# Tails in transfers of their own, rotated on DVE, and a new first order, in an attention kernel with two feed-forward layers behind it

## The chip, the cores and the metric

The kernel runs on one core of a Trainium2 chip. The metric is the device time of the whole program in microseconds (us). A change of 0.2% is 2.2 us here.

## The reference, cut to what matters

```python
def rotate(x):                       # q and k, [4, 8, 576, 64], float32
    x1, x2 = x[..., :32], x[..., 32:]
    return concatenate([x1 * cos - x2 * sin, x1 * sin + x2 * cos], axis=-1)
scores = matmul(rotate(q), rotate(k).T) / sqrt(64)
scores = scores - max(scores, axis=-1)
attn = exp(scores) / (sum(exp(scores)) + 1e-9)
x = matmul(attn, v)                  # heads side by side: [2304, 512]
x = (s * relu(x @ w_in) ** 2 + b) @ w_out          # 512 -> 2048 -> 512
h = x @ w2_in
out = (h * sigmoid(1.702 * h)) @ w2_out
```

## The kernel before, in words

The 32 heads are taken in 16 pairs. A head has 576 rows: 512 of them ("mains", NM = 4 tiles of 128) and 64 more ("tails"). The tails of the two heads of a pair share one tile, head 0 on partitions 0 to 63 and head 1 on 64 to 127. To keep float32 accuracy a matrix product is made of a high part (rounded to fp32r) and a low part (the rest), so each operand is split by ACT (high) and DVE (low).

A job is named kind, head and tile, and after the @ the pair: S01@2 is tile 1 of head 0 of pair 2. For each pair these jobs follow one another:

- load: SP issues the transfers of q and k into `raw` (L431 mains, L433 tails, which come as one transfer of [2, 64, 64] for q and one for k).
- rot: POOL rotates a head (L388 two products, L398 and L399 a difference and a sum), and adds one to `rotated`. A load waits until the rotation before it has read `raw`.
- prep: PE transposes the rotated head into PSUM (L679, L681). qk: ACT writes the high part (L781). klo: DVE writes the low part (L858).
- qcopy, kcopy: SP moves the parts between partitions (L456, L461). S00 of a pair with p > 0 waits for its kcopy.
- S, ST: PE makes a tile of scores (L579) and the tile of the tails (L594). max: DVE (L805, L811). exp: ACT (L713, L720).
- X, XQ, XT: PE transposes the exponentials (L605, L615, L631). hi: ACT. lo: DVE. PV: PE multiplies by V (L651), which takes V's parts from POOL (V, L518, and vlo, L522). eps, inv, IT, put, get, finish: the sums' reciprocals and the last scaling.

PE, ACT, DVE, POOL and SP each run their jobs strictly in the order of a list written out by hand: `PE_FIRST` and its like for about the first three pairs, then `PE_ORDER` and its like, repeated with a step of a pair. `FIRST_SLOTS` says which PSUM banks a job takes; a job whose bank is still to be read waits for its reader. The feed-forward layers follow (L956, L984).

Pair 0 has a path of its own. Its q and k go to `raw_0` (a part of buffer E), mains of head 0, tails, mains of head 1 (L483, L485, L487), and ACT issues the rotation tables' mains, their tails (L786, one transfer of [2, 64, 32] for each table) and the identity that PE transposes with (L787). DVE rotates the mains in four groups, q and k of head 0 and q and k of head 1 (`first_products` L405, two instructions; `first_sums` L416, L418); POOL rotates the tails in the same way. The first groups add to `first_rotated`, the tails to `first_tails`. Then `prep_first` (L666, L668) transposes, ACT makes the high parts (L771, L773), and DVE the low ones in `qk_first` (L840, L842). POOL starts rot0@1 after `first_rotated` has come to 4, which is all four groups.

Of the kernel before, what the change touches and what calls it, by code (L numbers as in the profile page):

```python
# [30 lines left out]
def fused_kernel(nc, q, k, v, w1_in, w1_out, w_s, w_b, w2_in, w2_out,  # L31
# [66 lines left out]
    SP_FIRST = order("load0@2 qcopy0@1 load1@2 kcopy0@1 qcopy1@1 kcopy1@1 load0@3 load1@3 qcopy0@2 qcopy1@2 kcopy0@2 "
                     "loadv0@1 kcopy1@2 load0@4 load1@4 qcopy0@3 qcopy1@3 load0@5 kcopy0@3 put@0 kcopy1@3 loadv1@1 "
                     "loadv0@2 qcopy0@4 get@0 kcopy0@4 load1@5 load0@6 put@1 loadv1@2 qcopy1@4 loadv0@3 get@1")  # L100
    FIRST_SLOTS = [0, 0, 0, 1, 3, 0, 2, 1, 3, 0, 5, 0, 3, 1, 2, 0, 1, 3, 1, 0, 3, 2, 1, 1, 3, 4, 5, 0, 3, 2, 0, 1, 4,
                   5, 7, 1, 0, 1, 2, 0, 3, 1, 0, 3, 2, 1, 0, 3, 0, 3, 2, 7, 2, 3, 0, 2, 6, 7, 2, 3, 0, 1, 7, 2, 0, 3,
# [1038 lines left out]
```

## Time and profile before

| | us |
|---|---|
| median of 3 runs | 1118.81 (1118.38 to 1119.59) |
| the profiled execution's own time | 1119.24 |
| its span | 1117.4 |
| PE busy in the span | 1090.4 |
| DVE, ACT, POOL busy | 553.5, 500.8, 247.4 |

The span is the time from the first to the last instruction in the trace, here 1.84 us less than that execution's own time. Matrix multiplications are pipelined, so that PE's busy time is not PE at its peak, but a stretch in which PE isn't busy is one in which nothing is computed there.

### The profile page before, as it was taken

What the parts mean: (1) busy time and instruction counts of PE and PEld (TensorE: products, weight loads), DVE (VectorE), ACT (ScalarE), POOL (GpSimd) and SP (SyncE); (2) the same over time, 40 slices, a digit from 0 to 9 for tenths busy, and PEclk for the clock granted to TensorE, in tenths of its full rate; (3) what the DMA queues carried; (4) which work ended last, traced back from release to release, by engine and by line L of the source; (5) the groups of instructions that cost most, each with busy time, mean ns of one, the idle gap of its engine ahead of it and who ended that gap; (6) DMA issues with size and microseconds to landing.
All of it is one profiled execution on the core that took longest, in us unless ns stands there. A gap on an engine that the chain in (4) does not pass through costs nothing.

```text
span 1117.4 us, 16936 instructions
## 1 busy us (share of the span) xinstructions
PE 1090.4 (98%) x6522; PEld 1036.1 (93%) x6522; DVE 553.5 (50%) x885; ACT 500.8 (45%) x1031; POOL 247.4 (22%) x276
## 2 busy tenths in 40 slices
PE   4899999999999999999999999999999999999998
PEld 4899999999999999999999999999999999999997
DVE  6888888898866333333333356532332323333222
ACT  4888788878755332232332345422322222222222
POOL 6878878895720000000000000000000000000000
PEclk9999999999999999999999999999999999999999
DMA  4555454553243100000000014200000000000000
GB/s 109 126 147 145 128 152 130 147 138 91 69 132 125 37 1 1 1 1 1 1 1 1 1 57 133 76 1 1 29 1 29 1 15 15 1 29 1 29 1 29
DMA packets 59187, 59.47 MB, mean 53 GB/s; under 512 B 13780, under 2 KB 46820, under 8 KB 59108
## 3 DMA queue, kind: packets, MB, share of 16 engines
q1 hardware_dynamic: 58272, 57.90, 18.6%
q8 instruction: 52, 0.85, 0.3%
q10 hardware_dynamic: 836, 0.49, 0.1%
q14 instruction: 27, 0.22, 0.1%
HBM read 35.88 MB, written 4.79 MB: 36 GB/s over the span
## 4 chain that ended last, share of the span: by engine, by line
PE 90%; DVE 4%; ACT 3%; DMA 1%; issue 1%; POOL 1%; SPq 0%; ACTq 0%; POOLq 0%; DVEq 0%
PE psum L956 36%; PE psum L984 36%; PE psum L651 7%; PE psum L605 4%; PE psum L579 4%; ACT E L713 2%; DVE negmax L805 1%; PE psum L681 1%; DVE osum L835 1%; DVE Xlo L815 1%; PE psum L615 0%; PE psum L631 0%; DMA sin<-in_k_sin_dram 0%; PE psum L679 0%; DVE QK L858 0%
## 5 line engine op out<-in xcount | busy, mean ns | idle before, releaser
L956 PE MATMUL psum<-xhi,Wlo 128*128 128x384 f32 x768 | 257.8, 336 | 0.0
L956 PE MATMUL psum<-xhi,Whi 128*128 128x384 f32 x768 | 257.6, 335 | 0.0
L956 PE MATMUL psum<-xlo,Whi 128*128 128x384 f32 x768 | 257.2, 335 | 0.0
L956 PEld LDWEIGHTS psum<-xhi,Whi 128*128 128x128 f32 x768 | 144.2, 188 | 4.2
L956 PEld LDWEIGHTS psum<-xlo,Whi 128*128 128x128 f32 x768 | 144.1, 188 | 4.1
L956 PEld LDWEIGHTS psum<-xhi,Wlo 128*128 128x128 f32 x768 | 144.1, 188 | 0.0
L937 DVE SCALAR_TENSOR_TENSOR glo<-act,sb_sb,ghi 128x384 fp32r<-128x384 f32 x96 | 59.4, 619 | 145.4 <-ACT ghi L924 145.4
L924 ACT ACTIVATE ghi<-act,sb_sb 128x384 fp32r<-128x384 f32 x96 | 59.2, 617 | 157.7 <-PE psum L984 150.3
L940 DVE TENSOR_TENSOR glo<-act,ghi 128x384 fp32r<-128x384 f32 x96 | 53.6, 559 | 152.0 <-ACT ghi L926 152.0
L984 PE MATMUL psum<-ghi,Whi 128*128 128x384 f32 x384 | 128.3, 334 | 0.0
L984 PE MATMUL psum<-glo,Whi 128*128 128x384 f32 x384 | 128.3, 334 | 0.0
L984 PE MATMUL psum<-ghi,Wlo 128*128 128x384 f32 x384 | 128.3, 334 | 0.0
L926 ACT CAST ghi<-act 128x384 fp32r<-128x384 f32 x96 | 49.3, 514 | 157.0 <-PE psum L984 157.0
L934 DVE TENSOR_TENSOR act<-psum,act 128x384 f32<-128x384 f32 x96 | 53.5, 558 | 124.1 <-ACT act L920 124.1
L984 PE MATMUL psum<-Wlo,ghi 128*128 128x512 f32 x288 | 113.9, 396 | 0.0
L984 PE MATMUL psum<-Whi,glo 128*128 128x512 f32 x288 | 113.7, 395 | 0.0
L984 PE MATMUL psum<-Whi,ghi 128*128 128x512 f32 x288 | 111.9, 389 | 0.0
L920 ACT ACTIVATE act<-psum 128x384 f32<-128x384 f32 x96 | 47.2, 492 | 129.6 <-PE psum L956 129.6
L713 ACT ACTIVATE E<-psum,negmax 128x576 f32<-128x576 f32 x128 | 94.7, 745 | 13.6 <-DVE negmax L805 13.3
L805 DVE TENSOR_REDUCE negmax<-psum 128x1 f32<-128x576 f32 x128 | 91.2, 752 | 14.7 <-PE psum L579 14.1
L932 DVE SCALAR_TENSOR_TENSOR act<-act,sb_sb 128x384 f32<-128x384 f32 x96 | 60.3, 628 | 76.4 <-ACT act L918 76.4
L579 PE MATMUL psum<-QK,Q 128*128 128x320 f32 (+1 forms) x512 | 86.3, 309 | 9.1 <-ACT E L713 6.9
(107 smaller groups left out, 1844.4 us busy)
## 6 DMA issues: line engine op xcount, KB each, us to landing
Q<-QK SPq DMA_DIRECT2D x60, 144.0 KB, 3.1
QK<-QK SPq DMA_DIRECT2D x30, 288.0 KB, 3.4
wraw<-in_moe_w_in_dram SPq DMA_DIRECT2D x32, 256.0 KB, 2.9
wraw<-in_moe_w_out_dram SPq DMA_DIRECT2D x32, 256.0 KB, 3.1
vraw<-in_v_dram SPq DMA_DIRECT2D x32, 128.0 KB, 2.3
raw<-in_q_dram SPq DMA_DIRECT2D x30, 128.0 KB, 2.9
raw<-in_k_dram SPq DMA_DIRECT2D x30, 128.0 KB, 2.8
inv_row<-inv_dram SPq DMA_DIRECT2D x16, 144.0 KB, 2.9
```

The source lines that it names most:

```text
L579: mm = pe.matmul(ps[:, a:b], Q[h][p % 2][:, at:at + P], QK[h][p % 2][:, part, c:c + b - a], start=part == 0, stop=part == 1)
L651: mm = pe.matmul(ps[:, a:b], V[h][:, j, :, :].rearrange("p a d -> p (a d)"), x, start=j == 0 and n == 0, stop=j == NM and n == 1, skip_gro ...
L713: act.activation(E[p % 2][:, j, h, :], row(banks("S", p, h, j), h), ACT.Exp, bias=negmax[p % 2][:, c:c + 1], accum_out=sums[p % 2][:, c:c ...
L805: dve.tensor_reduce(negmax[p % 2][:, c:c + 1], row(banks("S", p, h, j), h), AX_X, ALU.max, negate=True).then_inc(max_done, 1)
L924: act.activation(ghi[n % 2][:], a[:], ACT.Identity, bias=sb_sb[:, 1:2]).then_inc(g_hi, 1)
L926: act.copy(ghi[n % 2][:], a[:]).then_inc(g_hi, 1)
L932: dve.scalar_tensor_tensor(a[:], a[:], sb_sb[:, 0:1], a[:], ALU.mult, ALU.mult).then_inc(g_done, 1)
L934: dve.tensor_tensor(a[:], hps(n), a[:], ALU.mult).then_inc(g_done, 1)
L937: dve.scalar_tensor_tensor(glo[n % 2][:], a[:], sb_sb[:, 1:2], ghi[n % 2][:].bitcast(F32), ALU.add, ALU.subtract).then_inc(g_lo, 1)
L940: dve.tensor_tensor(glo[n % 2][:], a[:], ghi[n % 2][:].bitcast(F32), ALU.subtract).then_inc(g_lo, 1)
L956: mm = pe.matmul(hps(n), w[i][:, kt * P:(kt + 1) * P], x[C % 2][:, kt, :], start=kt == 0 and j == 0, stop=kt == KT - 1 and j == 2)
L984: mm = pe.matmul(dst, lhsT, rhs, start=i == 0 and j == 0, stop=i == NF - 1 and j == 2)
```

## The change

1. **Transfers.** The tails of pairs 0 and 1 (q and k) and the tails of the tables go as one transfer for each half of the partitions: 64 rows each, 16 transfers in place of 8. From pair 2 on the tails are as before.
2. **Who rotates the tails of pair 0.** DVE does, after head 0's q and k and before head 1's q. POOL's six instructions for it go, and so do `first_tails` and `tails_step`. `first_rotated` now counts five groups: q0, k0, tails, q1, k1. PE's `prep_first(0)` waits for 3 of them, `prep_first(1)` for 4 and 5. POOL's wait before rot0@1 is still for 4.
3. **Low parts.** `qk_first(0)` on DVE comes ahead of the group k1 (it was the first job of `DVE_FIRST`).
4. **ACT** loads its table and makes its first small exponential before it waits for the rotation tables.
5. **Orders.** All five first lists and the slots are new. On PE ST@0 comes before S02@0, prep0@1 before ST@0, X01@0 before S13@0, and prep0@3 and prep1@3 come ahead of PV0@0, where prep1@3 came after S03@2 and ST@2.

```diff
-    PE_FIRST = order("prep0@0 prep1@0 S00@0 S01@0 S02@0 prep0@1 S03@0 ST@0 S10@0 prep1@1 X00@0 S11@0 S12@0 S13@0 S00@1 "
-                     "prep0@2 S01@1 S02@1 S03@1 S10@1 prep1@2 S11@1 ST@1 XQ@0 XT@0 X01@0 X02@0 S12@1 S13@1 X03@0 IT@0 "
-                     "X10@0 X11@0 X12@0 X13@0 prep0@3 PV0@0 S00@2 S01@2 S02@2 S03@2 ST@2 prep1@3 S10@2 S11@2 S12@2 "
+    PE_FIRST = order("prep0@0 S00@0 S01@0 prep1@0 prep0@1 ST@0 S02@0 S03@0 S10@0 prep1@1 S11@0 S12@0 X00@0 X01@0 S13@0 "
+                     "S00@1 S01@1 S02@1 S03@1 prep0@2 prep1@2 X02@0 X03@0 S10@1 S11@1 ST@1 IT@0 XT@0 XQ@0 S12@1 "
+                     "prep0@3 X10@0 X11@0 X12@0 S13@1 X13@0 prep1@3 PV0@0 ST@2 S00@2 S01@2 S02@2 S03@2 S10@2 S11@2 "
...
+    ACT_FIRST = order("qk0@0 exp00@0 qk1@0 qk0@1 exp01@0 expT@0 exp02@0 qk1@1 exp03@0 exp10@0 hi00@0 hi01@0 exp11@0 "
...
+    DVE_FIRST = order("klo0@0 max00@0 max01@0 klo1@0 klo0@1 maxT@0 max02@0 max03@0 max10@0 klo1@1 max11@0 max12@0 "
...
+    POOL_FIRST = order("rot0@1 rot1@1 V0@0 rot0@2 rot1@2 eps@0 vlo0@0 rot0@3 rot1@3 V1@0 V0@1 vlo1@0 eps@1 rot0@4 rot1@4 "
...
+    SP_FIRST = order("load0@2 qcopy0@1 load1@2 kcopy0@1 qcopy1@1 kcopy1@1 load0@3 load1@3 loadv0@1 qcopy0@2 qcopy1@2 "
...
-                def tails(t, p):
-
-                    return t[2 * p:2 * p + 2, MAIN:S, :]
+                def tails(rows, t, p, apart):
+
+                    if apart:
+                        for h in range(2):
+                            yield rows[rows_of(h), :], t[2 * p + h, MAIN:S, :]
+                    else:
+                        yield rows, t[2 * p:2 * p + 2, MAIN:S, :]
...
-                            sp.dma_start(to[:, w, NM, :], tails(t, p)).then_inc(qk_in[h], 16)
+                            for dst, src in tails(to[:, w, NM, :], t, p, p == 1):
+                                sp.dma_start(dst, src).then_inc(qk_in[h], 16)
...
-                        pool.wait_ge(qk_in[h], (64 if h == 0 else 32) * p)
+                        pool.wait_ge(qk_in[h], 96 + 64 * (p - 1) if h == 0 else 32 * p)
...
-                pool.wait_ge(tab_tails_in, 32)
-                pool.wait_ge(first_tails_in, 32)
-                for w in range(2):
-                    first_products(pool, w, NM, NM + 1, slice(NM, NT), tails_step)
-                first_sums(pool, 4, NM, NM + 1, None, tails_step, first_tails)
+                pool.wait_ge(tab_tails_in, 64)

                 pool.wait_ge(first_rotated, 4)
...
                 def prep_first(h):
-                    pe.wait_ge(first_tails, 1)
...
-                        pe.wait_ge(first_rotated, 2 * h + w + 1)
+                        pe.wait_ge(first_rotated, 3 if h == 0 else 4 + w)
...
-                    act.dma_start(tab[:, NM, :], src[0:TAIL, NM, :].unsqueeze(0).broadcast_to([2, TAIL, HALF])).then_inc(tab_tails_in, 16)
+                    for h in range(2):
+                        act.dma_start(tab[rows_of(h), NM, :], src[0:TAIL, NM, :]).then_inc(tab_tails_in, 16)
                 act.dma_start(id_sb[:], ident).then_inc(id_in, 16)
+                act.wait_ge(cleared, 1)
+                act.activation(negmax[0][:], sums[0][:], ACT.Exp)
...
-                for n, (first, w) in enumerate(((0, 0), (0, 1), (NM + 1, 0), (NM + 1, 1))):
-                    dve.wait_ge(first_in[n], 16)
-                    first_products(dve, w, first, first + NM, slice(0, NM), first_step)
-                    first_sums(dve, 2 * n + 2, first, first + NM, w, first_step, first_rotated)
+                dve.wait_ge(first_in[0], 16)
+                first_tiles(0, 0, NM, (0,), slice(0, NM))
+                dve.wait_ge(first_in[1], 16)
+                first_tiles(1, 0, NM, (1,), slice(0, NM))
+                dve.wait_ge(tab_tails_in, 64)
+                dve.wait_ge(first_tails_in, 64)
+                first_tiles(2, NM, NM + 1, (0, 1), slice(NM, NT))
+                dve.wait_ge(first_in[2], 16)
+                first_tiles(4, NM + 1, TILES, (0,), slice(0, NM))
+                qk_first(0)
+                dve.wait_ge(first_in[3], 16)
+                first_tiles(5, NM + 1, TILES, (1,), slice(0, NM))
```

`first_tiles` makes the products of the groups that it is given and then their difference and sum, six instructions for the tails and four for each of the others.

## Rows read from the trace of the kernel before

**Rows 1.** The page's busy time of each engine, share of the span and instructions.
```profile
PE 1090.4 (98%) x6522; PEld 1036.1 (93%) x6522; DVE 553.5 (50%) x885; ACT 500.8 (45%) x1031; POOL 247.4 (22%) x276
```

**Rows 2.** Stretches: length, PE, PEld, DVE, ACT, POOL busy, clock, DMA share, GB/s.
```profile
12.00:26.00 14.00, 11.32 (x69) 10.12 (x69) 9.62 (x14) 9.00 (x19) 12.98 (x12) 1.00 0.28 73
26.00:29.00 3.00, 2.68 (x11) 2.38 (x11) 1.92 (x3) 1.94 (x5) 2.86 (x3) 0.51 0.82 197
29.00:45.00 16.00, 14.04 (x106) 12.74 (x105) 13.75 (x21) 14.13 (x33) 12.41 (x15) 0.99 0.64 159
45.00:90.00 45.00, 42.76 (x329) 40.31 (x329) 38.06 (x59) 34.72 (x79) 37.29 (x40) 1.00 0.48 121
```

**Rows 3.** The chain that ended last, from 0 to 60 us: start, length, what.
```profile
3.07 5.17 DMA sin<-in_k_sin_dram
...
8.47 1.93 POOL E L405 x4
```

**Rows 4.** The stretch 8.3 to 9.6 us, columns as in rows 2.
```profile
8.30:9.60 1.30, 0.00 (x0) 0.00 (x0) 1.27 (x4) 1.28 (x1) 1.13 (x3) 1.00 0.15 39
```

**Rows 5.** DMA issues in order of time, and line L442 by itself (ns).
```profile
1.67 1.36 ACTq L786 DMA_DIRECT2D cos<-in_k_cos_dram  x1
7.15 1.98 SPq L431 DMA_DIRECT2D raw<-in_q_dram  x1
L442 SPq DMA_DIRECT2D vraw<-in_v_dram x3: 493/528/802, 10.1 to 39.1; - x3
DMA to landing us min/median/max: 2.0/2.3/2.6
```

**Rows 6.** DVE's, then POOL's instructions in order of time: start, length, what.
```profile
5.24 0.42 DVE L405 TENSOR_TENSOR E<-E,cos 128x256 f32<-128x256 f32 x1
6.37 0.42 DVE L418 TENSOR_TENSOR E<-E 128x256 f32<-128x256 f32 x1
8.07 0.43 DVE L405 TENSOR_TENSOR E<-E,cos 128x256 f32<-128x256 f32 x1 [1.28 <-DMA E<-in_q_dram]
9.67 0.54 DVE L405 TENSOR_TENSOR E<-E,cos 128x256 f32<-128x256 f32 x1
10.13 0.54 DVE L405 TENSOR_TENSOR E<-E,sin 128x256 f32<-128x256 f32 x1
9.89 0.50 POOL L405 TENSOR_TENSOR E<-E,sin 128x64 f32<-128x64 f32 x1
10.95 0.63 POOL L418 TENSOR_TENSOR E<-E 128x128 f32<-128x128 f32 x1
```

**Rows 7.** PE's and DVE's instructions in order of time, from 11.8 us on.
```profile
11.83 0.45 PE L666 MATMUL psum<-id_sb,E 128*128 128x128 f32 x1 [11.83 <-POOL E L418]
14.90 0.76 DVE L842 TENSOR_TENSOR QK<-psum,QK 128x576 fp32r<-128x576 f32 x1
17.52 2.08 DVE L805 TENSOR_REDUCE negmax<-psum 128x1 f32<-128x576 f32 x3
20.39 1.30 PE L594 MATMUL psum<-QK,Q 128*128 128x256 f32 x10
23.84 0.82 DVE L858 SCALAR_TENSOR_TENSOR QK<-psum,qk_scale,QK 128x576 fp32r<-128x576 f32 x1 [0.20 <-ACT QK L781]
```

**Rows 8.** SP's, POOL's and PE's instructions around pair 3's rotation, in order of time.
```profile
16.79 0.33 SPq L431 DMA_DIRECT2D raw<-in_q_dram  x1
29.84 1.39 SPq L431 DMA_DIRECT2D raw<-in_q_dram  x1
21.56 1.55 POOL L388 TENSOR_TENSOR byc<-raw,cos 128x640 f32<-128x640 f32 x1 [0.64 <-DMA raw<-in_k_dram]
36.23 1.55 POOL L388 TENSOR_TENSOR byc<-raw,cos 128x640 f32<-128x640 f32 x1 [3.35 <-DMA raw<-in_k_dram]
45.18 0.74 POOL L399 TENSOR_TENSOR rot<-bys,byc 128x256 f32<-128x256 f32 x1
43.58 0.36 PE L651 MATMUL psum<-Xhi,V 128*128 128x256 f32 x1
```

More of the change, by code:

```diff
@@ L78, in fused_kernel @@
     BANK_ORDER = (6, 0, 7, 1, 2, 3, 4, 5)
-    PE_FIRST = order("prep0@0 prep1@0 S00@0 S01@0 S02@0 prep0@1 S03@0 ST@0 S10@0 prep1@1 X00@0 S11@0 S12@0 S13@0 S00@1 "
[4 rows of a table removed]
-    ACT_FIRST = order("qk0@0 qk1@0 exp00@0 exp01@0 qk0@1 exp02@0 exp03@0 qk1@1 expT@0 hi00@0 exp10@0 exp11@0 exp12@0 "
[5 rows of a table removed]
-    DVE_FIRST = order("klo0@0 klo1@0 max00@0 max01@0 max02@0 klo0@1 max03@0 maxT@0 max10@0 klo1@1 lo00@0 max11@0 "
[5 rows of a table removed]
-    POOL_FIRST = order("rot0@1 rot1@1 rot0@2 rot1@2 V0@0 eps@0 V1@0 vlo0@0 rot0@3 vlo1@0 rot1@3 eps@1 V0@1 vlo0@1 rot0@4 "
-                       "rot1@4 rot0@5 eps@2 V1@1 V0@2 vlo1@1 vlo0@2 rot1@5 finish@0 V1@2 vlo1@2 rot0@6 finish@1")
@@ L98, in fused_kernel @@
[L98 to L102, printed above, removed]
+    PE_FIRST = order("prep0@0 S00@0 S01@0 prep1@0 prep0@1 ST@0 S02@0 S03@0 S10@0 prep1@1 S11@0 S12@0 X00@0 X01@0 S13@0 "
[4 rows of a table added]
@@ new lines, in fused_kernel @@
+    ACT_FIRST = order("qk0@0 exp00@0 qk1@0 qk0@1 exp01@0 expT@0 exp02@0 qk1@1 exp03@0 exp10@0 hi00@0 hi01@0 exp11@0 "
[5 rows of a table added]
+    DVE_FIRST = order("klo0@0 max00@0 max01@0 klo1@0 klo0@1 maxT@0 max02@0 max03@0 max10@0 klo1@1 max11@0 max12@0 "
[5 rows of a table added]
+    POOL_FIRST = order("rot0@1 rot1@1 V0@0 rot0@2 rot1@2 eps@0 vlo0@0 rot0@3 rot1@3 V1@0 V0@1 vlo1@0 eps@1 rot0@4 rot1@4 "
+                       "V1@1 vlo0@1 vlo1@1 eps@2 rot0@5 rot1@5 V0@2 finish@0 V1@2 vlo0@2 vlo1@2 rot0@6 finish@1")
+    SP_FIRST = order("load0@2 qcopy0@1 load1@2 kcopy0@1 qcopy1@1 kcopy1@1 load0@3 load1@3 loadv0@1 qcopy0@2 qcopy1@2 "
+                     "kcopy0@2 load0@4 kcopy1@2 qcopy0@3 qcopy1@3 load1@4 kcopy0@3 kcopy1@3 loadv1@1 load0@5 put@0 "
+                     "qcopy0@4 qcopy1@4 loadv0@2 load1@5 get@0 loadv1@2 put@1 kcopy0@4 load0@6 load1@6 kcopy1@4 "
+                     "loadv0@3 get@1 qcopy0@5")
@@ L103, in fused_kernel @@
+    FIRST_SLOTS = [0, 1, 0, 0, 1, 2, 0, 3, 1, 2, 0, 2, 7, 2, 3, 0, 2, 1, 3, 0, 2, 1, 0, 1, 3, 2, 2, 3, 1, 2, 1, 7, 6,
+                   0, 2, 1, 1, 3, 1, 3, 0, 2, 1, 3, 0, 2, 1, 3, 0, 4, 1, 6, 7, 0, 1, 2, 0, 3, 2, 7, 6, 2, 0, 1, 2, 3,
                    1, 0, 2, 7, 6, 1, 0, 2, 1, 0]
@@ L197, in fused_kernel @@
         first_rotated = sem("first_rotated")
-        first_tails = sem("first_tails")
-        tails_step = sem("tails_step")
         first_t = sem("first_t")
@@ L484, in attention_sync @@
                 for w, t in enumerate((q_h, k_h)):
-                    sp.dma_start(group(raw_0, NM, NM + 1)[:, w, 0, :], tails(t, 0)).then_inc(first_tails_in, 16)
+                    for dst, src in tails(group(raw_0, NM, NM + 1)[:, w, 0, :], t, 0, True):
+                        sp.dma_start(dst, src).then_inc(first_tails_in, 16)
                 for w, t in enumerate((q_h, k_h)):
@@ L785, in attention_scalar @@
                 for tab, src in ((cos, k_cos), (sin, k_sin)):
-                    act.dma_start(tab[:, NM, :], src[0:TAIL, NM, :].unsqueeze(0).broadcast_to([2, TAIL, HALF])).then_inc(tab_tails_in, 16)
+                    for h in range(2):
+                        act.dma_start(tab[rows_of(h), NM, :], src[0:TAIL, NM, :]).then_inc(tab_tails_in, 16)
                 act.dma_start(id_sb[:], ident).then_inc(id_in, 16)
+                act.wait_ge(cleared, 1)
+                act.activation(negmax[0][:], sums[0][:], ACT.Exp)
                 act.wait_ge(tabs_in, 32)
-                act.wait_ge(tab_tails_in, 32)
+                act.wait_ge(tab_tails_in, 64)
                 for tab, twice in ((cos, cos_2), (sin, sin_2)):
                     act.copy(twice[:], tab[:, :, :].unsqueeze(2).broadcast_to([P, NT, 2, HALF])).then_inc(tabs_twice, 1)
-                act.wait_ge(cleared, 1)
-                act.activation(negmax[0][:], sums[0][:], ACT.Exp)
                 act.wait_ge(scale_set, 1)
@@ L855, in qk_low @@
                     if p == 0:
-                        return qk_first(h)
+                        return qk_first(1) if h == 1 else None
                     dve.wait_ge(qk_hi, 2 * p + h + 1)
@@ L863, in attention_vector, with first_tiles @@
                 dve.wait_ge(tabs_in, 32)
-                for n, (first, w) in enumerate(((0, 0), (0, 1), (NM + 1, 0), (NM + 1, 1))):
-                    dve.wait_ge(first_in[n], 16)
-                    first_products(dve, w, first, first + NM, slice(0, NM), first_step)
-                    first_sums(dve, 2 * n + 2, first, first + NM, w, first_step, first_rotated)
+                def first_tiles(n, first, end, ws, tab):
+                    for w in ws:
+                        first_products(dve, w, first, end, tab, first_step)
+                    first_sums(dve, 2 * n + 2 * len(ws), first, end, ws[0] if len(ws) == 1 else None, first_step, first_rotated)
+                dve.wait_ge(first_in[0], 16)
[10 more added lines that the diff above has]
+                first_tiles(5, NM + 1, TILES, (1,), slice(0, NM))
                 dve.wait_ge(cleared, 1)
```

24 rows, old and new, of tables (ACT_FIRST, DVE_FIRST, PE_FIRST) are left out of this document.

## The prediction, made before the change was run

> **What bounds the kernel now.** I read the page first: PE is busy 98% of the span, so the time is PE's work plus what PE stands idle [rows 1]. The change adds and removes no work on PE; it can only shift idle time, and there are 27.0 us of it (1117.4 - 1090.4). Next I read the busy time by stretches. PE starts at 11.83 [rows 7], idles 2.7 us from 12 to 26, 0.3 from 26 to 29, 2.0 from 29 to 45 and 2.2 from 45 to 90 [rows 2]. So 19 of the 27 us lie ahead of 90 us, and the change touches only that part. The granted clock matters too: it is 0.51 from 26 to 29, the level of 1.2 GHz, after PE had waited in the stretch before [rows 2]. Third, the chain of waits shows what holds the start: the tables' tails, issued at 3.07, land at 8.24, POOL takes them up at 8.47 [rows 3], and PE starts when POOL's L418, begun at 10.95 [rows 6], is done. Last, the timelines of POOL, SP and PE around 30 to 46 us, since the first order moves jobs there [rows 8].
>
> **The transfers.** From 8.3 to 9.6 us, with only the tails still in flight (pair 1's behind pair 0's), the DMA share is 0.15 at 39 GB/s [rows 4]: 2.4 of 16 engines. A transfer of [2, 64, ...] seems to run on about two engines. The nearest row for the new form is L442, V's tails, 64 rows from one head: issue 0.53, landing 2.3 us after the issue starts [rows 5]. In the new kernel SP issues two mains from 0.74 at 0.45 each and four tails at 0.53, the last from 3.2; ACT's last tail of a table also starts at about 3.2. Both land at about 5.5 to 6. Issues that took 1.36 and 1.98 [rows 5] could add up to 2 us; DVE has work until 6.8 [rows 6], which hides a landing at 6 and 0.8 us more.
>
> The row L442 speaks for the spread by itself. The Trainium skill, page "DMA: Bandwidth & Descriptors", section "Rules for kernel authors", says the opposite of what this change does: two transfers to disjoint halves of the partitions are not worth it, since they serialize on the same engines, and one should be used. By it the tails would land no sooner than 8.2; the trace has 2.3 us for a half and some 5 for the whole, so the row disagrees for this shape; rival E has that outcome.
>
> **The tails on DVE.** Six instructions of 64 or 128 columns. Below they cost nothing beyond the order (DVE waits 1.28 us for q1 anyway, up to 8.07 [rows 6]); above, six at the 0.42 of 256 columns, 2.5 us. Four of 256 columns take 1.5 us in a row (5.24 to 6.79 [rows 6]), and these have a quarter or half of the columns, so I take 1.1 us for the six. DVE goes 6.8 to 7.9, PE starts at about 8.0, **3.8 us earlier**. q1 is rotated from 7.9 to 9.4. In before DVE ended the first low parts at 15.66, 3.83 after PE's start [rows 7]; now 11.85. S00@0 can run then.
>
> **POOL against DVE.** This is where I think the lead is lost. POOL's rot0@1 waits for `first_rotated` 4, which was everything and is now only q1, at 9.4. Its data: four more issues stand ahead of its end on SP's queue (two tails of pair 0, two of its own), the last starts at about 7.1 to 8.1, and lands at 9.4 to 10.4. So rot0@1 starts at about 10.4, not 11.94, and the group k1, which comes after `qk_first(0)` at 11.85, runs beside it. In before DVE's instructions with two inputs in SBUF, which take 0.42 alone, take 0.54 and start every 0.46 while POOL rotates the tails; POOL's end at 10.39, DVE's at 10.21 and 10.67, so they alternate: 0.28 for DVE, 0.18 for POOL's 64 columns, and 0.31 for its 128 [rows 6]. Two bounds follow. If only a fixed 0.12 to 0.2 is lost, k1 takes 2.2 us and ends at 14.0. If each waits for the whole instruction of the other, k1's four instructions alternate with POOL's, of 1.5 us and twice about 0.8 (estimated for 320 columns from 0.74 for 256) [rows 8]: 11.9 to 12.2, 13.7 to 14.0, 14.8 to 15.1, 15.9 to 16.2; with another start of POOL the end is up to 17.1. Since POOL's turn grew from 0.18 to 0.31 as its columns doubled, I take 16.2. The Trainium skill, page "SBUF — State Buffer", section "Who interferes with whom", has it so: a VectorE instruction with two SBUF inputs and a GpSimd one that reads SBUF lock each other out for the whole instruction. By that rule k1 ends at 16.2 to 17.1, without it at 14.0; this trace shows it only for small POOL instructions.
>
> The first maximum is then made at 16.2 against 17.52 [rows 7], but DVE still owes the second head's low parts (1.5 us), which it had made by then. On this order: two maxima to 17.6, exp00 to 17.65, the second head's high parts on ACT to 18.9, its low parts to 19.85, klo0@1 to 20.6.
>
> **From there to the copies.** ST@0 takes 1.30 [rows 7], then S02, S03 and S10 (0.65 each) and prep1@1 (0.6): 23.7. With 0.75 for ACT and 0.8 for DVE, klo1@1 ends at 25.3, against 24.66 before [rows 7]. That is at full clock. But between 13.8 and 19.85 PE has little to do, and before the clock fell at 26 after a stretch with more work than that. At its start PE's transposes take 0.21 each up to about 15.4 and half of that later (the clock column shows 1.00 there, so I go by the durations), and from 26 to 29 the clock is 0.51: some 3 to 3.6 us at half rate each time. An estimate from these: 3.6 us at half rate from 19.85, which costs 1.8, klo1@1 at 27.1. The bounds are 25.3 and 27.1.
>
> **The load of pair 3 and prep1@3.** SP has load0@3 behind kcopy1@1, in both kernels. Before, it was issued at 29.84, and rot0@3 started at 36.23, after POOL had idled 3.35 us for it [rows 8]. From klo1@1's end to the issue it took 5.2 us, of which 0.75 for kcopy0@1 ahead of it, so 4.45 now: 29.75 or 31.55. From issue to rotation it is 6.4 us, or 4.8 as for pair 2 (16.79 to 21.56 [rows 8]): rot0@3 starts at 34.5 to 37.9. Both heads of pair 3 take 8.8 us (36.23 to 45.92, less 0.88 for vlo1@0 between them, which moves behind). Now prep1@3 stands ahead of PV0@0 on PE, and behind it waits everything PE has. Before, PE reached prep1@3 4.6 us after its rotation was done, and PV0@0 at 43.58 [rows 8]. The four combinations give rot1@3 done at 43.3, 44.9, 45.1 or 46.7 (29.75 or 31.55, plus 4.8 or 6.4, plus 8.8); with prep1@3 (0.6) PV0@0 starts at 43.9, 45.5, 45.7 or 47.3. Less the 0.6 of prep1@3, which is then done, PE is behind by -0.2, 1.4, 1.6 or 3.2 us. I take the mean, 1.5. From 45 us on PE is 95% busy [rows 2], so there is little to catch up with: of 2.2 us idle perhaps 0.1.
>
> The rest costs nothing: ACT's table load lies in its wait for the tables, and POOL's removed six instructions (3.1 us, 8.47 to 11.58 [rows 3, 6]) lay in a stretch where it now waits for pair 1's data.
>
> **The sum.** +1.5 - 0.1 = +1.4 us. Against the profiled execution 1119.24 + 1.4 = 1120.6; that execution was 0.4 above the median, and against the median 1118.81 the forecast is **1120.2**. A difference of 0.2%, 2.2 us, is about what a measurement tells from none.
>
> **The rivals.**
> - *A, the forecast*: the lead of 3.8 us goes to POOL and DVE locking each other and to the wait for prep1@3. -0.3 to +2.2 us. Chance 0.40.
> - *B, the same with the low clock and the slow landing*: +2.3 to +4, 1121.1 to 1122.8. It decides from klo1@1 ending after 26.1 where the landing takes 6.4. For it: the clock fell at 26 after less idle time. Against it: the landing may be 4.8. Chance 0.26.
> - *C, DVE isn't held up*: k1 ends at 14.0, 2.2 before A's, and all behind it moves with it at full clock: klo1@1 at 23.1, load0@3 at 27.6, PV0@0 at 41.8 to 43.4. PE leads by 0.8 to 2.4: 1116.4 to 1118.0. Chance 0.15, a third of it beyond 0.2%.
> - *D, the whole start is kept*: load0@3 is early enough that prep1@3 isn't late, and the new order loses nothing: -2.5 to -3.8, 1115.0 to 1116.3. Against it: POOL waited 3.35 us for this very load. Chance 0.13. It decides, beyond 0.2%, where klo1@1 ends before 23.3 with the landing in 4.8, before 21.7 with it in 6.4.
> - *E, the change of transfers does nothing* (the halves go on the same two engines one after the other: 4.6 us from issue to landing in place of 2.3, and two more issues): tails at 8.8, DVE through with them at 9.9, PE at 10.0, everything 2 us later than in A: about 1122. Chance 0.06.
>
> Slower by over 0.2%: B and most of E, and a little of A, 0.34. Faster: D, a third of C and errors in my hand count, 0.21. Within: 0.45. For 8 in 10 the range reaches from most of D to the middle of B: 1116.0 to 1122.4. A's own range is 1118.5 to 1121.0.
>
> **What would show it.** The transfers: DVE's wait before the tails is near nothing, and PE's first matmul starts at 8 to 8.5; at 10 or later would be E. The lock: the four instructions of k1 (L405, L416, L418) take about 1.5 us each or stand apart by that; at about 0.5 each in a row it is C. The clock: S tiles and ST@0 at half rate around 20 to 24. The load: POOL idle before rot0@3 on `raw`, and PE idle before L679 or L681 of prep1@3, just ahead of PV0@0, 1 to 4 us. The prediction is wrong if PE isn't idle there; then look whether load0@3 was issued before 28.

## The result, and the profile after

| | before | after |
|---|---|---|
| median, us (8 runs of each) | 1118.52 (1117.88 to 1119.59) | 1121.12 (1120.55 to 1122.4) |
| the profiled execution's own time | 1119.24 | 1121.25 |
| its span | 1117.4 | 1119.4 |

The ratio of the times is 1.0025, with an interval of 1.0014 to 1.0036: **2.6 us slower**, with 1.6 to 4.0 us as the interval: slower is clear, whether by more than 0.2% (2.2 us) is not quite. The forecast was 1120.2. By its account (+1.4) it was 1.2 us short, and the time lies at the lower end of rival B.

The page's busy times after, to be read against [rows 1]:

```profile
PE 1093.5 (98%) x6522; PEld 1037.7 (93%) x6522; DVE 556.9 (50%) x891; ACT 500.0 (45%) x1031; POOL 244.4 (22%) x270
```

PE has the same 6522 instructions and is busy 3.1 us longer, so it ran slower somewhere; its idle time is 25.9 us against 27.0. The sum is the 2.0 us of the span. Where they lie shows the busy time by stretches: first after, in the stretches of [rows 2] and then up to the first matmul of PV0@0 and from it on (columns as in rows 2):

```profile
12.00:26.00 14.00, 11.28 (x51) 9.91 (x51) 11.03 (x13) 5.02 (x11) 10.94 (x10) 1.00 0.32 78
26.00:29.00 3.00, 2.08 (x15) 1.88 (x16) 2.35 (x4) 2.26 (x6) 2.74 (x3) 1.00 0.46 98
29.00:45.00 16.00, 13.09 (x96) 11.21 (x95) 13.17 (x21) 14.52 (x34) 11.77 (x13) 1.00 0.65 154
45.00:90.00 45.00, 43.49 (x330) 40.59 (x328) 38.47 (x60) 34.48 (x79) 37.97 (x41) 1.00 0.49 127
...
8.06:46.43 38.37, 29.83 (x177) 25.74 (x178) 30.89 (x44) 24.25 (x54) 28.73 (x28) 1.00 0.52 123
...
46.43:1119.40 1072.97, 1063.65 (x6348) 1011.91 (x6346) 521.73 (x832) 473.51 (x973) 214.63 (x229) 1.00 0.18 50
```

The last two stretches for the kernel before, from PE's start to its PV0@0 and from there on:

```profile
11.83:43.58 31.75, 26.78 (x173) 24.00 (x173) 23.88 (x36) 23.80 (x54) 26.97 (x27) 0.95 0.51 127
...
43.58:1117.40 1073.82, 1063.62 (x6351) 1012.05 (x6350) 522.84 (x833) 474.81 (x974) 216.40 (x230) 1.00 0.18 50
```

PE starts 3.77 us earlier, but needs 38.37 us to PV0@0 in place of 31.75: 3.05 more busy (0.6 of it prep1@3, which now stands ahead; the rest is more time at half rate, by the durations below) and 3.57 more idle (8.54 against 4.97). So it comes to PV0@0 2.85 us late, and makes up 0.85 from there to the end. Between 12 and 26 us PE is as busy as before, 11.28 us, but for 51 instructions in place of 69.

DVE's instructions after, in order of time (start, length, what), which answer to [rows 6] and [rows 7]:

```profile
6.76 0.22 DVE L404 TENSOR_TENSOR E<-E,cos 128x64 f32<-128x64 f32 x1
...
11.81 1.67 DVE L404 TENSOR_TENSOR E<-E,cos 128x256 f32<-128x256 f32 x1
13.40 1.08 DVE L404 TENSOR_TENSOR E<-E,sin 128x256 f32<-128x256 f32 x1
14.52 0.97 DVE L415 TENSOR_TENSOR E<-E 128x256 f32<-128x256 f32 x1
15.41 1.48 DVE L417 TENSOR_TENSOR E<-E 128x256 f32<-128x256 f32 x1
16.82 1.41 DVE L807 TENSOR_REDUCE negmax<-psum 128x1 f32<-128x576 f32 x2
...
26.78 0.82 DVE L861 SCALAR_TENSOR_TENSOR QK<-psum,qk_scale,QK 128x576 fp32r<-128x576 f32 x1 [0.43 <-ACT QK L782]
```

POOL's after, the first ones and rot0@3:

```profile
10.15 1.54 POOL L387 TENSOR_TENSOR byc<-raw,cos 128x640 f32<-128x640 f32 x1 [8.61 <-DMA raw<-in_k_dram]
11.64 1.55 POOL L387 TENSOR_TENSOR bys<-raw,sin 128x640 f32<-128x640 f32 x1
13.28 0.93 POOL L397 TENSOR_TENSOR rot<-byc,bys 128x320 f32<-128x320 f32 x1
14.17 1.04 POOL L398 TENSOR_TENSOR rot<-bys,byc 128x320 f32<-128x320 f32 x1
15.35 1.26 POOL L387 TENSOR_TENSOR byc<-raw,cos 128x512 f32<-128x512 f32 x1
...
36.83 1.57 POOL L387 TENSOR_TENSOR byc<-raw,cos 128x640 f32<-128x640 f32 x1 [2.91 <-DMA raw<-in_k_dram]
```

The tails come at once (nothing waited for at 6.76, PE starts at 8.06). Then the lock: POOL's instructions end at 13.19, 14.21, 15.21 and 16.61, and the four of k1 on DVE, which take 0.42 alone, at 13.48, 14.48, 15.49 and 16.89, each 0.27 to 0.29 us behind POOL's. The first maximum is at 16.82, against 17.52, and klo1@1 ends at 27.60, against 24.66.

PE's after (the first bracket is what it waited for), and SP's issue of load0@3:

```profile
8.06 0.45 PE L667 MATMUL psum<-id_sb,E 128*128 128x128 f32 x1 [8.06 <-DVE E L417]
...
12.04 2.26 PE L580 MATMUL psum<-QK,Q 128*128 128x256 f32 x8 [1.61 <-DVE QK L844]
...
20.68 2.42 PE L595 MATMUL psum<-QK,Q 128*128 128x256 f32 x10 [0.81 <-DVE QK L844]
22.91 2.51 PE L580 MATMUL psum<-QK,Q 128*128 128x256 f32 x12
...
27.65 0.80 PE L580 MATMUL psum<-QK,Q 128*128 128x320 f32 x4 [0.92 <-DVE QK L861]
...
45.91 0.33 PE L680 MATMUL psum<-id_sb,rot 128*128 128x128 f32 x1 [0.41 <-POOL rot L398]
...
46.43 0.37 PE L652 MATMUL psum<-Xhi,V 128*128 128x256 f32 x1
```

```profile
31.12 0.58 SPq L434 DMA_DIRECT2D raw<-in_q_dram  x1
```

One thing fits the forecast's picture and one stands against it. ST@0 takes 2.42, where it took 1.30 before [rows 7], so PE runs at 1.2 GHz there, as the prediction's sign for the clock had it. But the wait ahead of prep1@3, which was to be 1 to 4 us, is 0.41. The other waits from 26 to 46 us are spread: 0.92 at 27.65 for klo1@1 and others of 0.16 to 1.06.

### The profile page after: what moved, and what is told of

Same layout as the page of the kernel before. It is cut to its first block, busy times and chain, and to the rows that moved or that the text cites. A ratio compares the mean times of both kernels' runs of the same rounds, so it can differ in the third digit from the quotient of the medians.

```text
span 1119.4 us, 16941 instructions
## 1 busy us (share of the span) xinstructions
PE 1093.5 (98%) x6522; PEld 1037.7 (93%) x6522; DVE 556.9 (50%) x891; ACT 500.0 (45%) x1031; POOL 244.4 (22%) x270
## 4 chain that ended last, share of the span: by engine, by line
PE 92%; DVE 3%; ACT 2%; POOL 1%; issue 1%; DMA 0%; ACTq 0%; POOLq 0%
PE psum L972 36%; PE psum L1000 36%; PE psum L652 8%; PE psum L606 4%; PE psum L580 4%; ACT E L714 2%; PE psum L682 1%; DVE negmax L807 1%; DVE osum L837 1%; PE psum L632 1%; PE psum L616 1%; PE psum L680 0%; PE psum L595 0%; DVE E L404 0%; POOL bys L387 0%
```

## The experiments

Twelve kernels were run, each beside the kernel before on the same chip. Times are medians; the difference is to the kernel before in the same comparison (1118.45 to 1118.70). Line numbers in rows are those of each kernel's own file.

| run | median (lowest to highest), us | difference | ratio, interval |
|---|---|---|---|
| 1. k1 ahead of the low parts | 1118.97 (1117.62 to 1119.44) | +0.5 | 1.0003, 0.9994 to 1.0012 |
| 2. POOL waits for k1 | 1119.56 (1119.32 to 1120.71) | +1.1 | 1.0011, 1.0002 to 1.002 |
| 3. the transfers alone | 1116.44 (1115.9 to 1118.23) | -2.0 | 0.9983, 0.9974 to 0.9992 |
| 4. prep1@3 behind PV0@0 | 1124.51 (1122.46 to 1124.86) | +6.1 | 1.0046, 1.0033 to 1.006 |
| 5. the old orders | 1121.21 (1120.89 to 1123.05) | +2.6 | 1.0025, 1.0015 to 1.0035 |
| 6. old orders, 1 and 2 together | 1117.02 (1116.84 to 1117.2) | -1.6 | 0.9985, 0.9976 to 0.9994 |
| 7. PE kept busy to 18 us | 1120.87 (1120.07 to 1122.19) | +2.3 | 1.0022, 1.0014 to 1.0031 |
| 8. the transfers undone | 1121.79 (1121.41 to 1122.92) | +3.2 | 1.003, 1.0018 to 1.0041 |
| 9. PE kept busy up to ST@0 | 1120.63 (1119.78 to 1122.1) | +2.1 | 1.0018, 1.0009 to 1.0027 |
| 10. old orders and k1 first | 1116.58 (1115.94 to 1117.0) | -1.9 | 0.9983, 0.9974 to 0.9992 |
| 11. as 3, tails apart for pairs 0 to 4 | 1116.56 (1116.06 to 1118.24) | -1.9 | 0.9984, 0.9975 to 0.9993 |
| 12. old orders, POOL waits for k1 | 1119.56 (1118.89 to 1120.62) | +0.9 | 1.0008, 0.9999 to 1.0017 |

Each interval reaches about 0.1%, 1.1 us, to either side. Those of run 1 and the change don't meet, nor do those of run 10 with run 1 or with run 5. Runs 2, 7, 8, 9 and 12 overlap with the kernel that they vary, and run 4 just does. What is said of the size of their effects rests on medians and on the rows of one profiled execution of each.

### Runs 1 and 2: taking k1 away from POOL's rotation

Run 1 puts the group k1 back ahead of the first low parts:

```diff
-                qk_first(0)
                 dve.wait_ge(first_in[3], 16)
                 first_tiles(5, NM + 1, TILES, (1,), slice(0, NM))
+                qk_first(0)
```

> The changed kernel with one thing undone: the group k1 on DVE comes before the first low parts again. Theory 1 (POOL and DVE keep each other out, so k1 beside rot0@1 ends at 16.8 and all behind it is late, at half clock): k1 now runs at 9.3 to about 11, at most its last instruction beside POOL's first (from 10.15); S00@0 starts at about 12.6 to 13, the first maximum at about 13.5 in place of 16.8, klo1@1 ends at 24 or earlier in place of 27.6, and the kernel is 2 to 4 us faster than the changed one (1117 to 1119). Theory 2 (the new order's waits for pair 3's rotation set the time): less than 1 us faster than the changed one, PE waits at prep1@3 for what is gained.

Run 2 leaves DVE's order and lets POOL start rot0@1 only behind k1:

```diff
-                pool.wait_ge(first_rotated, 4)
+                pool.wait_ge(first_rotated, 5)
```

> The changed kernel, but POOL waits for all five groups before rot0@1. Theory 1: k1's four instructions take 0.42 each again (1.5 us in all, done at 13.3), the first maximum is made at 13.3, but rot0@1 starts at 13.4 in place of 10.15, 3.2 us later, so prep0@1 (18.6 before) stays where it is and only what doesn't hang on it is early: 0.5 to 2 us faster than the changed kernel. If POOL's start doesn't slow k1 (theory 2), k1 still takes 5 us and the kernel is slower by 1 to 3 us, since the rotations are later.

Run 1 is 2.15 us faster than the change. Three of k1's instructions now take 0.42; the last still meets POOL's first. DVE's last one, the first maximum and klo1@1, and POOL's first, in run 1:

```profile
10.42 1.75 DVE L417 TENSOR_TENSOR E<-E 128x256 f32<-128x256 f32 x1
...
15.32 1.62 DVE L807 TENSOR_REDUCE negmax<-psum 128x1 f32<-128x576 f32 x2 [1.58 <-PE psum L580]
...
24.24 0.82 DVE L861 SCALAR_TENSOR_TENSOR QK<-psum,qk_scale,QK 128x576 fp32r<-128x576 f32 x1 [0.57 <-ACT QK L782]
```

```profile
10.15 1.75 POOL L387 TENSOR_TENSOR byc<-raw,cos 128x640 f32<-128x640 f32 x1 [8.60 <-DMA raw<-in_k_dram]
```

One instruction of 0.42 that starts 0.27 after POOL's becomes 1.75 and ends 0.27 behind it (12.17 against 11.90). With klo1@1 done at 25.06, PV0@0 comes at 43.94, though prep1@3 still stands ahead of it. PE's S00@0 and S01@0, ST@0 and the three tiles behind it, in run 1:

```profile
13.89 2.26 PE L580 MATMUL psum<-QK,Q 128*128 128x256 f32 x8 [3.47 <-DVE QK L844]
...
19.51 1.37 PE L595 MATMUL psum<-QK,Q 128*128 128x256 f32 x10 [1.31 <-DVE QK L844]
20.72 1.84 PE L580 MATMUL psum<-QK,Q 128*128 128x256 f32 x12
```

Not all of the gain is the lock. ST@0 starts 1.2 us earlier than in the change, and it and the tiles behind it are at full rate, 1.37 and 1.84 in place of 2.42 and 2.51, which is 1.7 us more. On the other side PE waits 3.47 us for the first low parts, so that S00@0 starts at 13.89 and not at 12.6 to 13 as expected, and klo1@1 ends at 25.06 and not at 24.

In run 2 k1 takes 0.42 for each instruction and the first maximum is at 13.44, 3.4 us before the change's. But rot0@1 starts at 13.65 in place of 10.15, and PE waits for it:

```profile
18.49 0.33 PE L680 MATMUL psum<-id_sb,rot 128*128 128x128 f32 x1 [2.46 <-POOL rot L398]
```

klo1@1 ends at 25.80 (27.60 in the change). ST@0 is at half rate there (2.43). So the lock is real and costs time, but taking it away by making POOL late gives back 1.6 us of it, no more.

### Runs 3, 8 and 11: the transfers

Run 3 is the kernel before with only the 16 transfers in halves: POOL still rotates the tails, and every order is as before.

```diff
-                    sp.dma_start(group(raw_0, NM, NM + 1)[:, w, 0, :], tails(t, 0)).then_inc(first_tails_in, 16)
+                    for dst, src in tails(group(raw_0, NM, NM + 1)[:, w, 0, :], t, 0, True):
+                        sp.dma_start(dst, src).then_inc(first_tails_in, 16)
...
-                    act.dma_start(tab[:, NM, :], src[0:TAIL, NM, :].unsqueeze(0).broadcast_to([2, TAIL, HALF])).then_inc(tab_tails_in, 16)
+                    for h in range(2):
+                        act.dma_start(tab[rows_of(h), NM, :], src[0:TAIL, NM, :]).then_inc(tab_tails_in, 16)
...
```

> The kernel before with only the 16 tails' transfers of 64 rows. If they spread over the DMA engines, the tails land at about 6 in place of 8.2, POOL rotates them at 6 to 8.5 (alternating with DVE), q1 is not waited for, PE starts at 9 to 9.5 in place of 11.83, and since all engines start 2 to 2.5 us earlier with the same orders, the kernel is 1.5 to 2.5 us faster than before (1116 to 1117). If halves serialize: PE starts at 11.5 or later and the time is that of before.

Run 8 is the change with the old single transfers; its diff is the reverse of this one, with the waits where the change has them. Run 11 is run 3 with `p == 1` made `1 <= p <= 4` for the pairs whose tails go apart.

> The changed kernel with the eight tails' transfers of before. Tails land at 8.2, DVE rotates them at 8.3 to 9.3, q1 after that to 10.8; PE starts at 9.5 in place of 8.06. POOL's rot0@1 then starts at 11 to 12 in place of 10.15, k1 runs beside it from about 13.3. All is 1 to 2 us later than in the changed kernel: 1 to 2 us slower (1122 to 1123). If the transfers are worth nothing here: the same time as the changed kernel.

> The kernel before with the tails' transfers apart for pairs 0 to 4 in place of 0 and 1. Loads of pairs 2 to 4 should land 0.5 to 1.5 us sooner, rot0@3 starts earlier. If PE's time hangs on them: 0.5 to 1 us faster than with pairs 0 and 1 alone (1115.5 to 1116). If not, as there, 1116.4, or a little more for two issues of 0.5 us more on SP's queue for each pair.

Run 3 gives 2.0 us, the largest gain of any one part. POOL's first instruction on the tails, PE's first and DVE's first maximum, in run 3:

```profile
6.03 0.32 POOL L405 TENSOR_TENSOR E<-E,cos 128x64 f32<-128x64 f32 x1 [4.48 <-DMA sin<-in_k_sin_dram]
```

```profile
9.17 0.44 PE L672 MATMUL psum<-id_sb,E 128*128 128x128 f32 x1 [9.17 <-POOL E L418]
```

```profile
15.05 2.08 DVE L812 TENSOR_REDUCE negmax<-psum 128x1 f32<-128x576 f32 x3
```

Against 8.47 [rows 3] for POOL, 11.83 and 17.52 [rows 7], these are 2.4, 2.7 and 2.5 us earlier. klo1@1 ends at 22.20 (24.66 before), load0@3 goes out at 27.40 (29.84 [rows 8]), and the span is 2.9 shorter, 1114.5. The lead is kept the whole way; the medians differ by 2.0. In run 8 DVE waits for the tables' tails, and PE starts 1.5 us after the change's 8.06, at 9.59:

```profile
8.28 0.23 DVE L404 TENSOR_TENSOR E<-E,cos 128x64 f32<-128x64 f32 x1 [1.42 <-DMA sin<-in_k_sin_dram]
```

The medians differ by only 0.7 us there (expected was 1 to 2). The profiled executions say something else: PV0@0 comes at 47.74 in place of 46.43, and the span is 1120.7 in place of 1119.4, so that 1.3 of the 1.5 us are still there at the end. Whether the transfers are worth 0.7 or 1.3 us inside the change isn't settled. Run 11 adds nothing to run 3 (the spans are both 1114.5), so tails of later pairs aren't waited for.

### Run 4: prep1@3 behind PV0@0

The theory was that PE loses its lead ahead of prep1@3. The lists keep the change's order but for this job and its readers on ACT and DVE, and the slots around it follow:

```diff
-                     "prep0@3 X10@0 X11@0 X12@0 S13@1 X13@0 prep1@3 PV0@0 ST@2 S00@2 S01@2 S02@2 S03@2 S10@2 S11@2 "
+                     "prep0@3 X10@0 X11@0 X12@0 S13@1 X13@0 PV0@0 prep1@3 ST@2 S00@2 S01@2 S02@2 S03@2 S10@2 S11@2 "
-                      "expT@1 hiT@0 hiQ@0 qk0@3 exp12@1 hi10@0 hi11@0 hi12@0 hi13@0 qk1@3 exp13@1 evac0@0 expT@2 "
+                      "expT@1 hiT@0 hiQ@0 qk0@3 exp12@1 hi10@0 hi11@0 hi12@0 hi13@0 exp13@1 evac0@0 qk1@3 expT@2 "
-                      "lo02@0 lo03@0 loT@0 max12@1 loQ@0 klo0@3 lo10@0 lo11@0 lo12@0 lo13@0 klo1@3 max13@1 sum0@0 "
+                      "lo02@0 lo03@0 loT@0 max12@1 loQ@0 klo0@3 lo10@0 lo11@0 lo12@0 lo13@0 max13@1 sum0@0 klo1@3 "
-                   0, 2, 1, 1, 3, 1, 3, 0, 2, 1, 3, 0, 2, 1, 3, 0, 4, 1, 6, 7, 0, 1, 2, 0, 3, 2, 7, 6, 2, 0, 1, 2, 3,
+                   0, 2, 1, 3, 1, 0, 3, 1, 2, 0, 3, 0, 2, 1, 3, 0, 4, 1, 6, 7, 0, 1, 2, 0, 3, 2, 7, 6, 2, 0, 1, 2, 3,
```

> The changed kernel with prep1@3 (and its high and low part) behind PV0@0, and the slots of ST@2, S01@2 to S03@2 changed so that no job waits for it sooner. The trace of the changed kernel has PE idle for only 0.41 us before prep1@3, so I expect 0.3 to 0.6 us faster, within what can be measured. The prediction's own step (PE is held 1 us or more by rot1@3) would want 1 us or more.

It was **3.4 us slower** than the change, where 0.3 to 0.6 us faster was expected. PE comes to PV0@0 at 46.60 all the same (46.43 in the change), after a wait for DVE's low parts. It then meets a new wait, and part of the stretch behind it is at half rate. PE's instructions, and the stretch 54 to 58 us, in run 4:

```profile
46.60 0.35 PE L652 MATMUL psum<-Xhi,V 128*128 128x256 f32 x1 [0.61 <-DVE Xlo L817]
...
56.14 3.21 PE L580 MATMUL psum<-QK,Q 128*128 128x320 f32 x12 [1.31 <-ACT E L714]
```

```profile
54.00:58.00 4.00, 2.67 (x13) 2.45 (x13) 2.19 (x4) 2.81 (x8) 3.78 (x5) 0.78 0.88 228
```

So prep1@3 isn't what makes PE late at PV0@0. What the move costs comes behind PV0@0, by these rows; no run took it apart.

### Runs 5, 6, 10 and 12: the orders

Run 5 is the change with all five first lists and slots of the kernel before. Run 10 adds run 1's edit, run 12 run 2's, and run 6 both.

> The changed kernel with the five first orders and the slots of before; transfers, tails on DVE, low parts ahead of k1 and POOL's wait for four stay. If the group k1 beside POOL is what costs, this order suffers more: prep1@0, ahead of S00@0, needs k1 (done at about 16.8), so S00@0 starts at about 17.5 in place of 15.89 before: 1 to 3 us slower than before (1119.5 to 1121.5). If the new orders are what costs, it is 2 to 3 us faster than before, like the transfers alone.

> The same with the old orders, k1 ahead of the low parts, and POOL waiting for all five groups, so that DVE's rotations never run beside POOL's. PE starts at 8.05, k1 is done at 10.8, S00@0 starts at about 12.1 (15.89 before), the first maximum at 13.7 (17.52), POOL's rot0@1 at 10.9 (11.94). If a start without that overlap is kept by the old orders: 2 to 3.8 us faster than before (1114.7 to 1116.5), at least as fast as the transfers alone. If POOL's chain of rotations and loads (1.1 us earlier) sets the gain: 1 us.

> The changed kernel with the old orders and k1 ahead of the low parts, POOL waiting for four groups. Only k1's last instruction meets POOL's first (10.15 to 11.7), which costs DVE 1.3 us and gives POOL 1.0 us against the run where it waited for five. If POOL's rotations set the pace there (PE waited 1.18 and 0.97 us for them), this is 0.3 to 1 us faster than that run (1116 to 1116.7); if DVE sets it, 0.5 to 1.3 us slower.

> The changed kernel with the old orders, low parts still ahead of k1, and POOL waiting for all five groups: it differs from the run with the old orders alone (1121.2) only in that POOL's rotation doesn't run beside k1. If the overlap is what costs there: k1's four instructions take 0.42 each and end at 13.4 in place of 16.9, the first maximum is made at about 16 in place of 19.7, POOL's rot0@1 starts at 13.5 in place of 10.2 and ends at 18.4, and the time is 2 to 3.5 us less (1117.7 to 1119.2). If it is the place of the low parts ahead of k1, whatever POOL does: 1120.5 to 1121.5 still.

With the old orders S00@0 stands behind prep1@0, and so behind k1. PE's wait for it and DVE's first maximum in run 5:

```profile
16.98 0.48 PE L666 MATMUL psum<-id_sb,E 128*128 128x128 f32 x1 [5.41 <-DVE E L416]
```

```profile
19.69 2.08 DVE L806 TENSOR_REDUCE negmax<-psum 128x1 f32<-128x576 f32 x3
```

The first maximum is 2.9 us behind the change's, yet klo1@1 ends at 26.84, 0.8 us before the change's, and the time is the same. DVE's rows in run 10, for comparison with run 1's:

```profile
10.53 1.76 DVE L416 TENSOR_TENSOR E<-E 128x256 f32<-128x256 f32 x1
...
15.33 0.76 DVE L806 TENSOR_REDUCE negmax<-psum 128x1 f32<-128x576 f32 x1
...
21.66 0.82 DVE L860 SCALAR_TENSOR_TENSOR QK<-psum,qk_scale,QK 128x576 fp32r<-128x576 f32 x1 [0.20 <-ACT QK L781]
```

The first maximum is at the same time in both (15.33, 15.32), but klo1@1 ends at 22.48 with the old orders and at 25.06 with the new ones, where the second head's preps stand behind S01@0 and its low parts behind two maxima. The medians differ by 2.4 us. PE's S00@0 to S02@0 in run 10, to be read against the 3.47 of run 1:

```profile
13.99 3.13 PE L579 MATMUL psum<-QK,Q 128*128 128x256 f32 x12 [0.33 <-DVE QK L843]
```

With the old orders PE makes prep1@0 (10.32 and 12.34) while it waits for the first low parts; with the new ones it stands idle and makes it from 15.95 on. So the second head's low parts are made at 13.88 to 15.41 in run 10 and at 17.84 to 19.37 in run 1, and ST@0 waits 1.31 us for them there. The corners, as differences to the kernel before:

| | old orders | new orders |
|---|---|---|
| k1 ahead of the low parts | -1.9 (run 10) | +0.5 (run 1) |
| low parts first, POOL waits for k1 | +0.9 (run 12) | +1.1 (run 2) |
| low parts first, POOL starts beside k1 | +2.6 (run 5) | +2.6 (the change) |

With k1 first, whether POOL waits for it too makes 0.4 us (run 6, 1117.02, against run 10, 1116.58), which is within the intervals. In run 6 all four instructions take 0.42, but PE then waits 1.18 and 0.97 us for POOL's rotation, so one lock of 1.3 us costs no more than the later start. Run 6 was expected to be at least as fast as run 3 and wasn't.

Run 12 came between what its two theories said. k1 is done at 13.41, 1.1 us later than in run 10, but rot0@1 starts at 13.73, 3.4 us later (10.32), and PE waits for it:

```profile
18.60 0.33 PE L679 MATMUL psum<-id_sb,rot 128*128 128x128 f32 x1 [1.23 <-POOL rot L397]
```

Together with a second wait of 0.99 behind it that puts klo1@1 at 25.16, against 22.48 in run 10 and 26.84 in run 5.

### Runs 7 and 9: the half rate

Both add transposes to PE that write the same values again, so that PE doesn't stand idle ahead of ST@0. Run 7 repeats prep1@0's q part seven times and puts 8 transposes ahead of S00@0. Run 9 also repeats its k part three times and puts 8 ahead of ST@0, as soon as DVE has read the bank. Its diff against run 7:

```diff
-                        for _ in range(7 if (h, w) == (1, 0) else 1):
+                        for _ in range(7 if (h, w) == (1, 0) else 3 if (h, w) == (1, 1) else 1):
...
+                    if p == 0:
+                        pe.wait_ge(low_read, 2)
+                        for n in range(8):
+                            pe.transpose(psum[2][:, ROW[0] + n % NM * P:ROW[0] + (n % NM + 1) * P], rotated_tile(NM + 1, NM + 1 + NM, n % NM, 0), id_sb[:])
...
```

> The changed kernel with 38 transposes more on PE, which write again what prep1@0 writes, in the idle time from 10.4 to 12 and 15.4 to 16.9 us; nothing else is changed. If PE's half rate up to 24 us costs (the low clock's share of the forecast): ST@0 takes 1.3 us in place of 2.42 and the three S tiles behind it 2.0 in place of 2.5, klo1@1 ends at 25.8 to 26.3 in place of 27.6, and the kernel is 1 to 2 us faster than the changed one. If the clock is of no account there, the time is the same.

> As the run before with repeated transposes, and more of them: the keys' part of prep1@0 three times in all, and eight ahead of ST@0, as soon as DVE has read the bank. The run before moved the half rate to 21 to 24.5 us and so didn't take it out of ST@0 and S02 to S10; here PE stands idle less than 0.6 us at a time up to ST@0. If it then stays at full rate: ST@0 takes 1.3 us, the three S tiles 2.0, klo1@1 ends at 25.5 to 26.3 (27.6 in the changed kernel), and the time falls by 1 to 2 us against the changed kernel if the half rate is worth that, or not at all if the load of pair 3 and DVE set it anyway.

ST@0 in run 7:

```profile
20.70 2.17 PE L595 MATMUL psum<-QK,Q 128*128 128x256 f32 x10 [1.37 <-DVE QK L850]
```

ST@0 and the three tiles behind it in run 9:

```profile
20.94 1.38 PE L600 MATMUL psum<-QK,Q 128*128 128x256 f32 x10
22.16 1.83 PE L581 MATMUL psum<-QK,Q 128*128 128x256 f32 x12
```

Run 7 is inconclusive for the price: PE was at full rate to 20 us, stood idle 0.86 and 1.37 us, and was at half rate from 21 to 24 all the same (granted clock 0.50). In run 9 both groups are at full rate: 1.38 and 1.83 in place of 2.42 and 2.51, 1.7 us less. klo1@1 ends at 26.50, 1.1 us before the change's, and the span is 1.1 shorter (1118.3). The medians differ by 0.5 (1120.63 against 1121.12) with runs spread over 2.3 us. So the half rate is worth 0.5 to 1.1 us here, less than the 1 to 2 expected; the medians' 0.5 is within the noise. It isn't the whole of the 2.6.

## Why the prediction was right or wrong

**The transfers** were right. The four halves of the tables land 2.2 and 2.6 us (medians) after their issue, as L442's did [rows 5], against 5.17 for the whole [rows 3]:

```profile
cos<-in_k_cos_dram ACTq DMA_DIRECT2D x2, 8.0 KB, 2.6
...
sin<-in_k_sin_dram ACTq DMA_DIRECT2D x2, 8.0 KB, 2.2
```

The mains that are issued behind them gain too: q's for pair 0 land 2.4 us after their issue in the median, against 3.7 before and 3.8 in run 8, and DVE's wait of 1.28 for q1 [rows 6] is gone. Run 3 shows that this alone is worth 2.0 us. The Trainium skill, page "DMA: Bandwidth & Descriptors", section "Rules for kernel authors", advises one transfer in place of two to the two halves of the partitions; for a transfer whose outermost dimension has size 2 the measurement decides against it, and the table of the same section has a second rule, that so small an outermost dimension keeps a transfer on that many engines, with which the 0.15 of [rows 4] and runs 3 and 8 agree. Rival E said about 1122, and with the old transfers run 8 came to 1121.8, but that is luck: E made everything 2 us later than A, and undoing the transfers moved PE's start by 1.5 and the median by 0.7, from a change that was itself 0.9 above the forecast.

**The tails on DVE**: 6.76 to 7.91, as forecast (1.1 us), PE at 8.06 (8.0), the first low parts done at 11.90 (11.85). The prediction didn't ask whether it is worth it. Run 3 leaves them on POOL and is the fastest of all with run 10, though PE starts 1.1 us later in it.

**POOL against DVE**: right in kind. The prediction's upper bound, each waiting for the whole instruction of the other, is what runs; the Trainium skill, page "SBUF — State Buffer", section "Who interferes with whom", has the same rule, and the 0.42 that became 1.75 agrees. The size was low: k1 ended at 16.89, in a range of 16.2 to 17.1 from which 16.2 was taken. That is 0.7 us.

**From there to the copies**: the bounds were 25.3 and 27.1, and klo1@1 ended at 27.60. By the forecast's own terms: 25.3, plus 0.7 for k1, plus the half rate, which is 1.7 by run 9's rows and which the forecast put at 1.8, is 27.7. Both terms were known; each was set at its low end or averaged.

**The load of pair 3 and prep1@3** is the step that failed as a cause. The prediction made PE's lateness wait ahead of prep1@3 for POOL, and so for load0@3. Its times held: the issue at 31.12 (29.75 to 31.55), rot0@3 at 36.83 (34.5 to 37.9), rot1@3 done at 45.85 (43.3 to 46.7), PV0@0 at 46.43 (43.9 to 47.3). But PE waited 0.41 us there, not 1 to 4, so that 2.4 of its 2.85 us were lost before, and without that place in the order it came no earlier (run 4). PE is late by itself: it follows klo1@1 as POOL does. klo1@1 is 2.9 us later than before and PV0@0 2.85; in run 1 it is 0.4 later (25.06) and PV0@0 0.36 (43.94). The sentence on how to tell, "The prediction is wrong if PE isn't idle there; then look whether load0@3 was issued before 28", offered only one other way, and it was neither. By that sentence the prediction is wrong in this step, though its time lies within its range. In part the times of the step held by luck: klo1@1 ended 0.5 us beyond the upper bound, and load0@3 followed it by 3.52 us, where 4.45 were reckoned.

**The sum.** Less the 0.6 of prep1@3, PE is behind by 2.25 us where "the mean, 1.5" was taken over four combinations, two of which left the half rate out. The rest of the span gave back 0.25 in the same account, and the profiled executions differ by 2.0 us, still in A's range, the medians by 2.6. So it is the first half of A, the lock, with B's conditions, and not A's wait ahead of prep1@3: klo1@1 after 26.1 and PE at 1.2 GHz, while the landing took 5.7 us from issue to rotation (31.12 to 36.83), between the two that were offered. B began at +2.3.

**C and D.** C was that DVE isn't held up. Run 2 makes it so with a price, and ends at 1119.6. D's argument against itself, that POOL waited 3.35 us for load0@3, doesn't stop a lead: in runs 3 and 10 one of 2.2 to 2.4 us goes through load0@3 (27.40 and 27.64 against 29.84) to the end. With k1 first and the orders left alone the change is faster than before by 1.9 us (run 10).

**What the change is made of**, then, by differences to the kernel before: 2.0 us gained by the transfers (run 3); nothing that could be measured by DVE's rotation of the tails and ACT's earlier table load (run 10 against run 3); 4.5 us lost by the low parts ahead of k1 with the old orders (run 10 to run 5), where k1 is done at 16.92 in place of 12.29. When POOL waits for k1, 1.7 of the 4.5 come back (run 12). The other 2.8 are k1's 1.1 us and POOL's later start together; what the lock alone costs no run shows, since none has the low parts first, POOL at 10.2 and no lock. The new orders lose nothing on top of it (run 5 against the change), since they start S00@0 without k1, but cost 2.4 us where k1 is early. For that the rows show prep1@0 no longer in PE's wait for the first low parts, and klo1@1 later by 2.6 us; no run moved one job of them alone, so the cause within the orders stays open.

The version to keep is the kernel before with the transfers in halves (run 3), 1116.44 against 1118.45; runs 6, 10 and 11 are the same within their intervals.

## What to carry to other kernels

Follow a lead to the last job that needs it before adding to it: here the transfers were worth 2.0 us, and a reordering made to use them earlier lost 4.5. Ahead of an instruction of DVE with two inputs in SBUF look at what POOL runs at that time: here such an instruction lasted until POOL's was done. Holding POOL back gave 1.6 and 1.7 us; moving DVE's instructions ahead of POOL's start gave 2.1 and 4.5, with all that came with it. And where two terms of a forecast have both come true elsewhere in the same trace (a full lock, a half rate after idle time), take them together, not the mean of having them and not.
